# RWKV-style decay attention, an MLP and routed experts on one core: decay products as a tree

## The reference

```
# attention: B=4, H=8, S=768, D=48
for t in range(S):
    cur = einsum('bhd,bhe->bhde', u * k[t], v[t])
    y[t] = einsum('bhd,bhde->bhe', r[t], state + cur)
    state = w[t][..., None] * state + einsum('bhd,bhe->bhde', k[t], v[t])
# MLP on 3072 tokens of 384 values
h = x @ w_in;  g = max(h, 0) + alpha * min(h, 0);  x = g @ w_out
# 8 experts, each token goes to the one with the highest gate
y = gate * (relu(x @ w1[e]) @ w2[e])
```

## Time and profile before

| | |
|---|---|
| median of 3 runs | 994.05 us (992.16 to 994.26) |
| span of the profiled execution | 990.5 us |
| what lies around it (median less span) | 3.5 us |
| PE busy | 816.2 us, 82% |
| DVE busy | 662.0 us, 67% |
| POOL busy | 459.6 us, 46% |
| ACT busy | 396.4 us, 40% |
| scans of the decay (L866) | 96, 88.5 us |
| reciprocals of the decay (L869) | 96, 87.9 us |

### The profile page before, as it was taken

How to read it: one execution, slowest core, us unless ns; L and a number is a source line. 1 busy time by engine, 2 the same in 40 slices (tenths; PEclk the granted TensorE clock), 3 DMA queues, 4 the chain that set the end, 5 groups by cost and what they waited for, 6 DMA issues and landing times.

```text
span 990.5 us, 18765 instructions
## 1 busy us (share of the span) xinstructions
PE 816.2 (82%) x6295; PEld 511.8 (52%) x6296; DVE 662.0 (67%) x1187; ACT 396.4 (40%) x666; POOL 459.6 (46%) x433
## 2 busy tenths in 40 slices
PE   3468788798887797978789788898499999999993
PEld 0354465366456346536545645655155655655651
DVE  8788878979977987897897898753333333333330
ACT  2544544454444453544445445363122222222220
POOL 7416755657765675765665577573101011101100
PEclk9788989998999999989989899999699999999997
DMA  8456217206315322620730632379544413344110
GB/s 255 185 154 171 76 63 226 88 1 231 105 41 184 117 76 73 221 86 2 244 99 34 197 104 76 115 259 344 201 169 173 152 48 103 115 158 170 32 47 13
DMA packets 43372, 128.96 MB, mean 130 GB/s; under 512 B 5632, under 2 KB 26784, under 8 KB 41504
## 3 DMA queue, kind: packets, MB, share of 16 engines
q1 hardware_dynamic: 30656, 105.03, 31.3%
q10 hardware_dynamic: 9120, 12.74, 4.7%
q0 software_dynamic: 3520, 10.17, 2.7%
HBM read 84.92 MB, written 43.78 MB: 130 GB/s over the span
## 4 chain that ended last, share of the span: by engine, by line
PE 42%; DVE 20%; issue 14%; POOL 14%; DMA 7%; ACT 3%; SPq 0%; DVEq 0%; POOLq 0%; ACTq 0%
DVE prod L866 5%; DMA arena<-expert_split 4%; POOL gl L564 4%; PE bank L1355 3%; PE bank L1557 3%; PE bank L1558 3%; PE bank L1559 3%; PE bank L1524 3%; PE bank L1526 3%; PE bank L1525 3%; PE bank L1446 3%; PE bank L1447 3%; PE bank L1448 2%; DVE inv L869 2%; POOL arena L536 2%
## 5 line engine op out<-in xcount | busy, mean ns | idle before, releaser
L1432 PE MATMUL bank<-xh,arena 128*128 128x384 f16 (+1 forms) x528 | 142.4, 299 | 68.3 <-DVE gf L1147 63.9
L564 POOL TENSOR_TENSOR gl<-gf,gh 128x384 f16<-128x384 f32 x128 | 120.4, 943 | 147.1 <-ACT gh L756 146.8
L586 POOL DMA_INDIRECT out_dram<-shared,dest x28 | 27.6, 986 | 257.3 <-DVE shared L1248 257.3
L1433 PE MATMUL bank<-xl,arena 128*128 128x384 f16 (+1 forms) x528 | 142.5, 299 | 0.0
L1446 PE MATMUL bank<-arena,gh 128*128 128x392 f16 x384 | 130.3, 339 | 5.9 <-POOL gl L564 5.9
L756 ACT ACTIVATE gh<-gf 128x384 f16<-128x384 f32 x128 | 66.4, 520 | 169.4 <-DVE gf L1147 166.3
L1447 PE MATMUL bank<-arena,gh 128*128 128x392 f16 x384 | 129.7, 338 | 0.0
L1448 PE MATMUL bank<-arena,gl 128*128 128x392 f16 x384 | 128.9, 336 | 0.0
L536 POOL TENSOR_TENSOR arena<-arena 128x768 f16<-128x768 f32 x64 | 112.3, 1759 | 0.7 <-ACT arena L702 0.7
L1432 PEld LDWEIGHTS bank<-xh,arena 128*128 128x128 f16 x528 | 54.3, 103 | 101.0 <-DVE gf L1147 71.0
L866 DVE TENSOR_TENSOR_SCAN prod<-rkw_sb 128x128 f32<-128x128 f32 x96 | 88.5, 974 | 18.6 <-POOL shared L502 12.5
(11 more groups left out here) (181 smaller groups left out, 1913.2 us busy)
## 6 DMA issues: line engine op xcount, KB each, us to landing
arena<-w_exp_dram SPq DMA_DIRECT2D x32, 768.0 KB, 5.6
expert_split<-arena SPq DMA_DIRECT2D x32, 768.0 KB, 4.2
arena<-expert_split SPq DMA_DIRECT2D x8, 3072.0 KB, 10.6
rkw_sb<-rkw_dram SPq DMA_DIRECT2D x64, 144.0 KB, 3.2
route_rows<-pad_rows ACTq DMA_DIRECT2D x8, 788.0 KB, 11.6
shared<-route_rows ACTq DMA_DIRECT2D x31, 197.0 KB, 2.8
rkw_sb<-rkw_dram SPq DMA_DIRECT2D x64, 72.0 KB, 4.0
v_sb<-v_dram SPq DMA_DIRECT2D x8, 576.0 KB, 7.9
```

Of the source, the lines that this page charges most:

```text
L564: pool.tensor_tensor(gl[:, f % 4, :], gf[:, f % 4, :], gh[:, f % 4, :], ALU.subtract).then_inc(gl_done, 1)
L1432: pe.matmul(at, wih[:, k, fs], xh[:, k, lo:hi], start=(k == 0), stop=False)
L1433: pe.matmul(at, wih[:, k, fs], xl[:, k, lo:hi], start=False, stop=False)
```

## The change

The running products are built as a tree. pair holds the products of two neighbouring w (192 values a pair of heads), quad the products of four (96 values). The three scans of a pair run over quad and so give every fourth value of P, stored with a step of four. One reciprocal gives inv at these places. The values between follow by multiplication: P at two steps past a fourth from P and pair, inv two steps before from inv and pair, and then in the same way the odd ones from w. The twelve pieces stay at the same f (the list is now PREP_AT) but are cut in another way: stage 0 has pair, quad and the scans, stage 1 the reciprocal and the first two products, stage 2 the last two. A new semaphore, prep_step, orders them. One semaphore, decay_done, takes the place of scan_done and inv_done; it rises at the end of stage 2, and both load_w on SP and kt on POOL wait for it.

```diff
-        RECIP_AT = [0, 1, 2, 3, 3, 4, 5, 6, 7, 8, 8, 9]
+        PREP_AT = [0, 1, 2, 3, 3, 4, 5, 6, 7, 8, 8, 9]
...
             def load_w(b, half, p, first):
                 if not first:
-                    sp.wait_ge(scan_done, NP * (2 * b + half) + p - 1)
+                    sp.wait_ge(decay_done, NP * (2 * b + half) + p - 1)
...
             def prep_qk(g, p):
                 n = NP * g + p
-                pool.wait_ge(inv_done, n + 1)
+                pool.wait_ge(decay_done, n + 1)
...
-            def prep(b, half, p, c):
+            def prep(b, half, p, stage):
                 n = NP * (2 * b + half) + p
-                if c == 0:
+                step = lambda k: dve.wait_ge(prep_step, 6 * n + k)
...
+                if stage == 0:
                     dve.wait_ge(w_arrived[p % 2], 32 * (2 * (2 * b + half) + p // 2 + 1))
                     if not (isinstance(n, int) and n < 2):
                         dve.wait_ge(prep_done, n - 1)
+                    dve.tensor_tensor(pairs[:, :, :].rearrange("p j r -> p (j r)"), w_pairs[:, :, 0], w_pairs[:, :, 1],
+                                      ALU.mult).then_inc(prep_step, 1)
+                    step(1)
+                    dve.tensor_tensor(quad[:, :], pairs[:, :, 0], pairs[:, :, 1], ALU.mult).then_inc(prep_step, 1)
+                    step(2)
                     for i in range(NC):
-                        w = rkw_sb[:, p % 2, 2, i * C:(i + 1) * C]
-                        last = dve.tensor_tensor_scan(prod[:, p, i, 1:C + 1], w, w, G, ALU.mult, ALU.bypass)
-                    last.then_inc(scan_done, 1)
-                    dve.wait_ge(scan_done, n + 1)
-                last = dve.reciprocal(inv[:, p % 2, c * C:(c + 1) * C], prod[:, p, c, 1:C + 1])
-                if c == NC - 1:
-                    last.then_inc(inv_done, 1)
+                        w = quad[:, i * (C // 4):(i + 1) * (C // 4)]
+                        last = dve.tensor_tensor_scan(from_1[:, i, :, 3], w, w, G, ALU.mult, ALU.bypass)
+                    last.then_inc(prep_step, 1)
+                elif stage == 1:
+                    step(3)
+                    dve.reciprocal(inv_4[:, :, :, 3], from_1[:, :, :, 3]).then_inc(prep_step, 1)
+                    dve.tensor_tensor(from_0[:, :, :, 2], from_0[:, :, :, 0], chunked[:, :, :, 0], ALU.mult
+                                      ).then_inc(prep_step, 1)
+                    step(4)
+                    dve.tensor_tensor(inv_4[:, :, :, 1], inv_4[:, :, :, 3], chunked[:, :, :, 1], ALU.mult
+                                      ).then_inc(prep_step, 1)
+                else:
+                    step(5)
+                    dve.tensor_tensor(from_0_by_2[:, :, :, 1], from_0_by_2[:, :, :, 0], w_chunked[:, :, :, 0], ALU.mult)
+                    step(6)
+                    dve.tensor_tensor(inv_2[:, :, 0], inv_2[:, :, 1], w_pairs[:, :, 1], ALU.mult).then_inc(decay_done, 1)
```

More of the change, by code:

```diff
@@ L107, in build @@
         inv = sb("inv", [128, 2, HALF], F32)
+        pair = sb("pair", [128, HALF // 2], F32)
+        quad = sb("quad", [128, HALF // 4], F32)
         qt = sb("qt", [128, 2, HALF], F32)
@@ L246, in build @@
         unit_lo = sem("unit_lo")
-        scan_done = sem("scan_done")
-        inv_done = sem("inv_done")
+        prep_step = sem("prep_step")
+        decay_done = sem("decay_done")
         pend_done = sem("pend_done")
@@ L855, in _ @@
             dve.wait_ge(dve_const, 4)
-            def prep(b, half, p, c):
+            def prep(b, half, p, stage):
                 n = NP * (2 * b + half) + p
-                if c == 0:
+                step = lambda k: dve.wait_ge(prep_step, 6 * n + k)
+                w_pairs = rkw_sb[:, p % 2, 2, :].rearrange("p (j r) -> p j r", r=2)
+                pairs = pair[:, :].rearrange("p (j r) -> p j r", r=2)
+                chunked = pair[:, :].rearrange("p (c j r) -> p c j r", c=NC, r=2)
+                w_chunked = rkw_sb[:, p % 2, 2, :].rearrange("p (c j r) -> p c j r", c=NC, r=2)
+                from_0 = prod[:, p, :, 0:C].rearrange("p c (j r) -> p c j r", r=4)
+                from_0_by_2 = prod[:, p, :, 0:C].rearrange("p c (j r) -> p c j r", r=2)
+                from_1 = prod[:, p, :, 1:C + 1].rearrange("p c (j r) -> p c j r", r=4)
+                inv_4 = inv[:, p % 2, :].rearrange("p (c j r) -> p c j r", c=NC, r=4)
+                inv_2 = inv[:, p % 2, :].rearrange("p (j r) -> p j r", r=2)
+                if stage == 0:
                     dve.wait_ge(w_arrived[p % 2], 32 * (2 * (2 * b + half) + p // 2 + 1))
@@ L894, in all_prep @@
             def all_prep(p):
-                for c in range(NC):
-                    prep(0, 0, p, c)
+                for stage in range(3):
+                    prep(0, 0, p, stage)
             all_prep(0)
@@ L1152, in mlp @@
                         continue
-                    for piece, at in enumerate(RECIP_AT):
+                    for piece, at in enumerate(PREP_AT):
                         if f == at:
-                            prep(nb, nh, piece // NC, piece % NC)
+                            prep(nb, nh, piece // 3, piece % 3)
                     if f == 5:
```

## The result

| | before | after |
|---|---|---|
| median | 993.1 us (10 runs, 989.9 to 999.6) | 1001.28 us (10 runs, 999.0 to 1003.0) |
| ratio to before, 95% interval | | 1.0078 [1.0059, 1.0096] |
| span of the profiled execution | 990.5 us | 997.3 us |
| DVE busy | 662.0 us | 663.8 us |
| POOL busy | 459.6 us | 451.1 us |

The forecast was slower, 1007 us in a range of 976 to 1030. The direction and the mechanism came out. The size did not: +13 us was forecast, +6.8 was measured on the spans of the two profiled executions and +8.2 on the medians.

The account below looks back on a forecast made before the run. No engine bounds it throughout; DVE paces seven of eight MLP stages, so neg(9)'s start counts. Half-batches 4 x 2.4 + 3 x 1.6 = 14.4, prologue -1: 990.5 + 13 = 1003.5, plus 3.5 gives 1007 us, range 976 to 1030.

Parts of the forecast that it names:

- The mechanism: Beside POOL: a DVE operation with two SBUF inputs pays up to one whole POOL operation, 0.9 to 1.65 us.
- Rival (a): MLP stages: DVE keeps the port through a burst, so the change is faster, -28 us to 966; chance 0.18.
- Rival (b): Decay work: strides put the six products at 0.44 us each, +15 us on the forecast, 1022; chance 0.14.
- The own durations: Decay work unhindered: 2.8 us a pair against 3.65 for the old, saving 0.85 us a pair.
- 3.5 us added on top as launch and end: Whole run: the median shown, 994.05, lies 3.5 us above the profiled span, added to 1003.5 for 1007.
- prologue: Before the first neg(0): only the last pair's decay work gets the 0.85 us unhindered saving, -1 us.
- neg(9), g = 0, 2, 4: Half-batches with w there at once: old scans ran free, so neg(9) starts 2.4 us later in each.
- neg(9), g = 1, 3, 5: Half-batches of the kind walked, where w lands late: neg(9) starts 1.6 us later in each.
- rest of the seven half-batches: After neg(9): PE works almost without a gap from hidden(12), so nothing was added, 0 us.
- The walk: Half-batch at 317.82, followed from f=0 to neg(9) with POOL's blocks: neg(9) at 359.3 instead of 357.71, +1.6 us.
- f=2: Walked half-batch: product behind L536 to 328.2, gl until 329.05, second product 329.3, neg(3) at 329.2.
- rival (c): Ties at gl (f=1, 2, 6) go to DVE half the time: 17 us off, 990 to 995; chance 0.13.

Follow-up runs that it names:

- experiment 1: Kernel before, with only the unused second input of the three scans read from PSUM instead of SBUF; ratio to before 0.9554.
- experiment 5: Kernel before, with one scan of 387 elements a pair instead of three of 128, second input in SBUF; ratio to before 0.9671.
- experiment 7: Changed kernel, with the second inputs of all nine two-input decay operations from PSUM (decay products wrong); ratio to before 0.9256.
- experiment 8: Changed kernel, with POOL's unit_low cut from 768 to 32 columns and DVE's instructions the same; ratio to before 0.9658.
- experiment 11: Kernel before, with load_w waiting for the end of a pair's reciprocals instead of its scans; ratio to before 0.9999.
- experiment 2: Changed kernel, with the unused second input of the three short scans read from PSUM; ratio to before 0.9872.
- experiment 3: Kernel before, full scans kept, but inv built by the tree (one reciprocal of 96, three products); ratio to before 0.9966.
- experiment 9: Kernel before, with the scans' dummy input in PSUM, one reciprocal of 96 and three products with w from PSUM; ratio to before 0.9391.
- experiment 10: Kernel before, with a single scan, second input in PSUM, one reciprocal of 96 and three products with w from PSUM; ratio to before 0.9402.
- experiment 4: Kernel before, with the running products built as a tree and three full reciprocals kept; ratio to before 1.0584.
- experiment 6: Kernel before, with one scan of 387 elements a pair instead of three, second input in PSUM; ratio to before 0.9496.

## Why the prediction was right, and where its size was off

**The mechanism was right.** A two-input operation pays for a POOL operation whatever its own length: experiments 1, 5, 7 and 8 each move the block and leave DVE's arithmetic nearly as it was, and the time follows. Experiment 1 is the cleanest of them, since it moves one operand and nothing else. Rival (a), a burst that keeps the port, is refuted for the MLP stage by POOL's rows above: DVE gets in between two POOL operations and no more. Rival (b), heavy strides, is refuted: quad and L888, with steps of two and four, take 0.26 us alone, and in experiment 7 254 and 274 ns, against a bound of 0.44. (L891 shows 0.32 alone, but starts 0.11 before L888 ends.) For steps of four float32 values, those of L888 and L891, the page "Advanced Engine Details and Errata" of the Trainium skill (Memory Cachelines) has a penalty. The trace shows next to nothing of it here.

**The own durations were right**: forecast 0.36, 0.26, 0.20 and 0.74 us, measured 0.34, 0.26, 0.2 (205 ns) and 0.75.

**The sum was off by 6 us**, 13 against 6.8. (The 3.5 us added on top as launch and end were also too many: the executions of the result lie 1.7 to 1.8 above their own spans; the rest was that the profiled execution was quicker than the median.) The terms, from the starts of neg(0) and of neg(9) in each half-batch of the two profiled executions:

| term | forecast us | measured us |
|---|---|---|
| prologue (start of the first neg(0): 75.3, now 72.0) | -1 | -3.3 |
| neg(9), g = 0, 2, 4 | +2.4 each | +1.7, +1.3, +1.3 |
| neg(9), g = 1, 3, 5 (w late before) | +1.6 each | -0.1, +0.4, +0.4 |
| neg(9), g = 6 | +2.4 | +3.3 |
| rest of the seven half-batches | 0 | +2.4 |
| last half-batch and experts (345.3, now 344.7) | 0 | -0.6 |

(The rows sum to +6.8.) The walk's own term is further off than the sum: seven half-batches, +8.3 against +14.4, and 2.1 of the 8.3 are a late w in g = 6 that the forecast had at 0. That leaves some 6 of 14. The terms put at -1 and 0 partly made up for it, which is luck. The walk through g = 3, as distances from neg(0):

| | neg(1) | neg(4) | neg(6) | neg(9) |
|---|---|---|---|---|
| before | 6.6 | 16.5 | 26.3 | 39.9 |
| forecast | 5.8 | 17.4 | 26.5 | 41.5 |
| after | 5.4 | 16.8 | 25.6 | 40.2 |

*The ties.* The step that was mis-sized is "f=2: ... product 328.2; gl until 329.05, product 329.3". It let POOL win every tie at gl. In the trace gl(2) came only at 330.30, while the second product started at 330.18 and ran free, 0.34 us. Of the three ties that rival (c) named (f=1, 2, 6), this one went to DVE: L891 was blocked at f=1 (1.02 us, above) and at f=6 (0.99 us). So a third of rival (c) came true, some 0.8 us in this half-batch out of the 1.3 that were missing, and the same in g = 1 to 6 (neg(2) to neg(3) takes 2.0 us in each). The rest is small: w came 3.0 us after neg(0) instead of 3.3, f=5 took 0.2 less than walked (7.2, not 7.45), f=6 to 8 took 0.4 less (14.6, not 15.0), and f=3 took 0.5 more (6.55, not 6.05).

*The two kinds.* The walk was made for one half-batch and carried to the others by adding 0.8 where w is early. To neg(9) the kernel before needs 36.8 us with w on time and 39.8 with w late, the changed one 38.1 (g = 2, 4) and 40.2. So like with like the change costs 1.3 with w on time, forecast 2.4, and 0.4 with w late, forecast 1.6. But which half-batches find w late changes from profile to profile: g = 1, 3, 5 before, g = 3, 5, 6 after, g = 3, 5 in experiment 11. And g = 1 after needs 39.7 though w is there: POOL's gl(0) starts 2.30 us behind neg(0), in g = 2 2.63, and so catches the three scans (2.65 us instead of 0.46). A third of a microsecond decides over one and a half, and a walk through one half-batch cannot give that.

*g = 6* was of the early kind before; in the profile after it waits for w:

```profile
571.87 0.36 DVE L876 TENSOR_TENSOR pair<-rkw_sb 128x192 f32<-128x192 f32 x1 [0.72 <-DMA rkw_sb<-rkw_dram]
```

Its +3.3 is the 1.3 of an early half-batch and some 2 of the late w. Experiment 11, with the late release alone, shows no such wait in g = 6 (nor in g = 1) and no loss of time, so the release does not explain it by itself. It stays open which transfer held it.

*The prologue.* The forecast counted 0.85 for the last pair only. The measured -3.3 looks like what all four pairs would give (4 x 0.85 = 3.4), but other runs speak against it. Experiment 1, which shortens no operation, starts its first neg(0) at 71.8, 3.5 early; experiment 8, with the changed kernel's DVE program, starts it at 74.7, only 0.7 early. So this term moves by some 3 us for reasons that were not found.

*The rest of the half-batches* was put at 0 and came to +2.4. PE's granted clock goes with it. Between neg(9) and neg(15), where PE catches up after its wait for gf(9), the clock is at its full level throughout in four of the seven half-batches before and in two after (means 0.95 and 0.90 of full speed), and PE is busy there for 88.8 us instead of 86.9. In the half-batch of the walk the first matmul of hidden(12) takes 0.34 us before and 0.50 after (above). No experiment separates this from the rest.

*Not foreseen at all* was a dearer neg: 608 ns in the mean instead of 575, over 128 of them 4.2 us. It is in the last section. Experiments 2, 3 and 7 to 10 have it as well, and no run takes it away alone.

**What of the listed signs came.** Nine two-input operations far above their free values: yes, except L888, L895 and L897 (311, 479, 370 ns), which often find POOL idle. The scans were to be "a fraction shorter in sum"; they take half (88.5 to 44.5). PE's wait at 10.5 to 11.5 us: 10.6. neg(9) 1.5 to 2.5 later: no, 0.35 in that half-batch and 1.2 in the mean of the seven (8.3 / 7). POOL's operations longer by less than 0.2: yes. An idle DVE before pair at f=5 ended by a DMA: no, POOL's khat ended it.

## What to carry to other kernels

Where DVE and POOL both work, count DVE's operations with two inputs in SBUF before their elements: cutting the work into more and shorter ones can cost more than it saves (three to nine here). Look for a second input that is a dummy, a constant or a copy that another engine can put into PSUM; moving one unused operand was worth 4.5% here, more than the whole redesign of the arithmetic. When walking a timeline, do not give every tie to the same side; count them, and state what the time is if some fall the other way (here one of three did).

## What the runs showed of the hardware that was not expected

- neg reads PSUM and has one tensor input, yet its duration depends on what DVE ran before it: 0.52 us behind a reciprocal (324.44 and 334.28 in the earlier trace rows), 0.58 to 0.59 behind a scan, 0.60 to 0.61 behind a product or a low part (337.00 above), 0.62 after a wait. In the kernels whose stages end in a reciprocal (before, 1, 4, 5, 6) its mean is 574 to 575 ns, in those that end in a product (after, 2, 3, 7 to 10) 608 or 609. Why is not known.
- The scan's price beside its length, unblocked: 32 elements 205 ns, 128 elements 400, 387 elements 951. That is near 2.1 ns an element, where a product takes about 1 (96 elements 254 ns, 192 elements 348).
- Taking a block away in one place raises it in another: with the scans free, ql goes from 925 to 1094 ns in experiment 1, and in experiment 2 the product behind the reciprocal from 311 to 550 (the changed kernel's value against experiment 2's).
